# Linear attention and two expert layers on one core: an opening program of its own for the first three chunks, with native fp32 products and the low parts of the weights on GpSimd

## The reference

```python
# r, k, v, w: 4 x 8 x 768 x 48
for t in range(S):
    cur = einsum('bhd,bhe->bhde', u[None] * kt, vt)
    y[:, :, t] = einsum('bhd,bhde->bhe', rt, state + cur)
    state = wt[:, :, :, None] * state + einsum('bhd,bhe->bhde', kt, vt)
x = y.transpose(0, 2, 1, 3).reshape(3072, 384)
# first expert, 384 -> 1024 -> 384
h = x @ w_in
e = exp(h - max(h)); sm = e / (sum(e) + 1e-09)
solu = h * sm
ln = (solu - mean(solu)) / sqrt(var(solu) + 1e-06) * g_ln
x = ln @ w_out
# second expert, 384 -> 2048 -> 384
h = x @ w_in2
out = maximum(0.01 * h, h) @ w_out2
```

## Time and profile before

| | us |
|---|---|
| median of 3 runs | 826.4 (826.23 to 827.62) |
| the profiled execution's own time | 825.48 |
| its span, first to last instruction | 823.7 |
| TensorE busy | 786.2 (95%) |
| VectorE busy | 521.3 (63%) |
| ScalarE busy | 338.8 (41%) |
| GpSimd busy | 196.7 (24%) |

### The profile page before, as it was taken

The page is one execution under the profiler, slowest core; times in us unless marked ns, Lnnn a source line. Parts: engine busy times, 40 slices in busy tenths (PEclk is TensorE's granted clock), DMA queues, the critical chain, the costliest instruction groups (busy, mean ns, idle before and its releaser), DMA issues.

```text
span 823.7 us, 11957 instructions
## 1 busy us (share of the span) xinstructions
PE 786.2 (95%) x4570; PEld 746.2 (91%) x4570; DVE 521.3 (63%) x1068; ACT 338.8 (41%) x652; POOL 196.7 (24%) x216
## 2 busy tenths in 40 slices
PE   2877999999999999999999999999999999999996
PEld 2655999999999999999999999999999999999996
DVE  7778776576575676667665765666765775553332
ACT  3335644344433444434434444335443444334332
POOL 4477823113111221121221131122131121000000
PEclk9976899999999999999999999999999999999999
DMA  7772211203202302203202122113112030000000
GB/s 193 248 228 58 58 30 29 58 2 87 58 1 58 87 1 58 58 1 88 58 1 58 28 61 58 29 29 87 29 30 58 1 87 30 1 1 29 1 0 32
DMA packets 18847, 43.50 MB, mean 53 GB/s; under 512 B 2272, under 2 KB 14688, under 8 KB 18400
## 3 DMA queue, kind: packets, MB, share of 16 engines
q1 hardware_dynamic: 14736, 33.24, 16.5%
q10 hardware_dynamic: 4048, 9.44, 3.3%
HBM read 37.95 MB, written 4.72 MB: 52 GB/s over the span
## 4 chain that ended last, share of the span: by engine, by line
PE 85%; DVE 0%; ACT 0%; issue 0%; ACTq 0%
PE BANKS L964 60%; PE MISC L964 21%; PE BANKS L1075 2%; PE MISC L994 1%; PE MISC L987 1%; DVE Rraw L863 0%; DVE RL L869 0%; ACT RH L633 0%; ACT Rraw L626 0%; DVE X2L L875 0%; ACT X2H L638 0%; ACT OUT L644 0%; DVE A L745 0%; DVE nmean L817 0%; ACTq L248 0%
## 5 line engine op out<-in xcount | busy, mean ns | idle before, releaser
L626 ACT ACTIVATE Rraw<-BANKS 128x384 f32<-128x384 f32 x128 | 62.9, 492 | 239.5 <-PE BANKS L964 237.8
L863 DVE TENSOR_TENSOR Rraw<-BANKS,Rraw 128x384 f32<-128x384 f32 x128 | 71.3, 557 | 133.5 <-ACT Rraw L626 133.0
L964 PE MATMUL BANKS<-RH,W4H 128*128 128x384 f32 x384 | 138.6, 361 | 0.9 <-DVE RL L869 0.8
L964 PE MATMUL BANKS<-X2H,W3H 128*128 128x384 f32 x384 | 130.4, 339 | 0.2 <-DVE X2L L875 0.2
L964 PE MATMUL BANKS<-X2L,W3H 128*128 128x384 f32 x384 | 129.1, 336 | 0.0
L964 PE MATMUL BANKS<-RL,W4H 128*128 128x384 f32 x384 | 129.1, 336 | 0.0
L964 PE MATMUL BANKS<-X2H,W3L 128*128 128x384 f32 x384 | 129.0, 336 | 0.0
L964 PE MATMUL BANKS<-RH,W4L 128*128 128x384 f32 x384 | 129.0, 336 | 0.0
L633 ACT ACTIVATE RH<-Rraw 128x384 fp32r<-128x384 f32 x128 | 67.1, 524 | 73.2 <-DVE Rraw L863 73.2
L436 POOL TENSOR_TENSOR ke<-att 112x512 f32<-112x512 f32 x24 | 29.5, 1230 | 255.3 <-DVE att L739 255.3
L735 DVE RECIPROCAL ki<-att 112x128 f32<-112x128 f32 x96 | 90.1, 941 | 0.0
(11 more groups left out here) (117 smaller groups left out, 1509.3 us busy)
## 6 DMA issues: line engine op xcount, KB each, us to landing
att<-rkw SPq DMA_DIRECT2D x48, 288.0 KB, 4.9
rtok<-r_tok SPq DMA_DIRECT2D x24, 192.0 KB, 4.5
ktok<-k_tok SPq DMA_DIRECT2D x24, 192.0 KB, 4.6
vtok<-v_tok SPq DMA_DIRECT2D x24, 192.0 KB, 4.7
out<-OUT SPq DMA_DIRECT2D x8, 576.0 KB, 5.6
W3raw<-w_in ACTq DMA_DIRECT2D x1, 3072.0 KB, 11.2
W4raw<-w_out ACTq DMA_DIRECT2D x1, 3072.0 KB, 24.3
W1raw<-w_in ACTq DMA_DIRECT2D x1, 1536.0 KB, 9.5
```

Of the source, the lines that this page charges most:

```text
L626: nc.scalar.activation(Rraw[:, fp % 2, :], PR[fp % 2][:, 0:ST], ACT.Copy, scale=0.01).then_inc(act_slope, 1)
L863: nc.vector.tensor_tensor(Rraw[:, fp % 2, :], PR[fp % 2][:, 0:ST], Rraw[:, fp % 2, :], ALU.max).then_inc(dve_relu, 1)
L964: return nc.tensor.matmul(dst, lhsT, rhs, start=start, stop=stop, skip_group_check=True)
```

## The change

- Three chunks get a program of their own, written out engine by engine; LEAD stays 28, but only 24 items (chunks 0 to 2) run ahead of the second expert's first stage. Items 25 to 52 are spread over that stage's 16 steps (1 or 2 a step); before, its steps carried items 37 to 52.
- Inputs of chunks 0 to 2 are loaded at once: chunk 2's into `att2`, tokens of chunks 1 and 2 into `tok12`, chunk 2's masked scores into `A2`, all in the space of W4H, which is not filled yet. ScalarE issues the loads of W1, W3, W2 at once and W4 after chunk 2's keys.
- The first expert of these chunks is computed in native fp32: X (ScalarE's copy alone) by W1raw, six products of 512 columns a chunk; its second half as W2raw by the transposed rows, which ScalarE copies with the gain as scale, 24 products of 128 columns a chunk, chunk by chunk. The GpSimd multiplication of W2 by the gain is gone; in later M1 steps the gain is the scale of ScalarE's high part and of VectorE's RL.
- Masks are made for two pairs at once; keys and queries of chunk 0 are handed over in two halves. The floor of the scan is read from PSUM for these chunks. VectorE and GpSimd share the first clearing of `att`.
- All low parts are made by GpSimd, in groups of 768 columns (4, 4, 8 and 8 groups for W1 to W4); W3 and the first group of W4 in the opening, the rest of W4, W1 and W2 in the first stage of the second expert. TensorE waits for each group of W3 and W4 by itself, for W1 at chunk 3's expert, for W2 at the second M1.

```diff
-def batch_steps(last):
+def batch_steps(last, opening=False):
...
+    for k, so, f, fp in out:
+        if opening and fp <= STEPS:
+            done = [CPS * SLOTS + (F1 + LEAD - CPS * SLOTS + F2) * j // F2 for j in (f, f + 1)]
+        else:
+            done = [fp + LEAD - 1, fp + LEAD]
+        listed.append((k, so, f, fp, [slot_of(i) for i in range(done[0] + 1, done[1] + 1)]))
...
+            load_T(0, 0)
             load_tok(0, 0)
             sp.dma_start(ub[:, :], u.partition_broadcast(CH)).then_inc(ld_u, 16)
-            load_T(0, 1)
-            for i in range(1, LEAD + 1):
-                item(0, *slot_of(i))
...
+            for m in (1, 2):
+                load_T(0, m)
+                load_tok(0, m)
+            load_tok(0, 3)
+            load_T(0, 4)
+            load_T(0, 3)
...
+            def low_part(w, g):
+                pool.wait_ge(split_hi[w], g + 1)
+                if w == 0:
+                    pool.wait_ge(pe_h, 2 * CPS)
+                if w == 1:
+                    pool.wait_ge(pe_cons, F1)
+                nc.gpsimd.tensor_tensor(group(los[w], w, g), group(raws[w], w, g),
+                                        group(his[w], w, g).bitcast(F32), ALU.subtract).then_inc(split_lo[w], 1)
...
             def body(b, last, item=item):
...
+                    if opening(b, kind, so):
+                        if f % 2 == 0 and f // 2 + 1 < GROUPS[3]:
+                            low_part(3, f // 2 + 1)
+                        if f < GROUPS[0]:
+                            low_part(0, f)
+                        if F1 <= f < F1 + GROUPS[1]:
+                            low_part(1, f - F1)
...
+            def take_ln(m):
+
+                wait(act, pe_m1, m)
+                for f in range(F1):
+                    wait(act, pe_lnT, m * 2 + f // 4 + 1)
+                    nc.scalar.activation(first_ln[:, f, :], ln_bank(m, f // 4)[:, f % 4 * CH:(f % 4 + 1) * CH],
+                                         ACT.Identity,
+                                         scale=gain[:, f:f + 1]).then_inc(act_lnT, 1)
...
+            take_x(0, 2)
+            normalise(0, 0)
+            exp_rows(0, 1)
+            take_ln(0)
+            normalise(0, 1)
+            exp_rows(0, 2)
+            for g in range(2, 4):
+                high_part(2, g)
+            take_ln(1)
+            normalise(0, 2)
+            for g in range(4, 6):
+                high_part(2, g)
+            part_heads(0, 3)
+            for g in range(6, 8):
+                high_part(2, g)
+            take_ln(2)
+            take_range(0, 3)
+            for g in range(2):
+                high_part(3, g)
+            take_x2(0, 0)
+            for g in range(4):
+                high_part(0, g)
...
+            def first_expert(m, halves=(0, 1)):
+
+                pe.wait_ge(act_x, m + 1)
...
+                for n in halves:
+                    for k in range(KM):
+                        last = mm(hidden(0, m)[:, n * 512:(n + 1) * 512], X[:, k, :], w1[:, k, n * 512:(n + 1) * 512],
+                                  k == 0, k == KM - 1)
+                    last.then_inc(pe_h, 1)
...
+            def first_out(m):
...
+                for f in range(F1):
+                    pe.wait_ge(act_lnT, m * F1 + f + 1)
+                    for k in range(KM):
+                        last = mm(ACC[k][:, m * CH:(m + 1) * CH], w2[:, f, k * 128:(k + 1) * 128], first_ln[:, f, :],
+                                  m == 0 and f == 0, f == F1 - 1)
...
+            first_scores(0, range(PAIRS))
+            first_attend(0, (0, 1))
+            first_keys(0)
+            first_attend(0, (2, 3))
+            first_state(0)
+            first_transposes(0)
+            first_expert(0, (0,))
+            first_scores(1, range(PAIRS))
+            first_keys(1)
+            first_attend(1, range(PAIRS))
+            first_state(1)
+            first_scores(2, range(PAIRS))
+            first_expert(0, (1,))
+            first_transposes(1)
+            first_keys(2)
+            first_attend(2, range(PAIRS))
+            first_state(2)
+            first_expert(1)
+            first_transposes(2)
+            first_rows(0)
+            first_expert(2)
+            first_out(0)
+            for m in (1, 2):
+                first_rows(m)
+                first_out(m)
```

More of the change, by code:

```diff
@@ L185, in build, with part, queries, keys @@
         plan["top"] = end
+        def part(x, b, m):
+            return att2[:, x, :, :] if first(b, m) and m == 2 else att[:, m % 2, x, :, :]
+        def queries(b, m):
+            return part(0, b, m)
+        def keys(b, m):
+            return part(1, b, m)
+        def decays(b, m):
+            return part(2, b, m)
+        def masked(b, m):
+            return A2 if first(b, m) and m == 2 else A
+        def tokens(x, b, m):
+            return tok12[m - 1][:, x, :] if first(b, m) and m > 0 else (rtok, ktok, vtok)[x][:, :]
         w1r = [t[:, :].rearrange("p (k n) -> p k n", k=KM) for t in (W1H, W1L)]
@@ L370, in body @@
             def body(b, last, item=item, first_row=0):
-                for kind, so, f, fp, m, s in batch_steps(last):
-                    item(b, m, s)
+                for kind, so, f, fp, items in batch_steps(last, isinstance(b, int) and b == 0):
+                    for m, s in items:
+                        item(b, m, s)
                     if kind == "M1" and f == 3:
@@ L1060, in item, with attend @@
                     transpose_y(b, m)
-                if s == 8 and not (first(b, m) and m < CPS - 1):
+                if s == 8:
                     expert_in(b, m)
+            def attend(b, m, a, at):
+                inter = m % CPB > 0
+                if inter:
+                    if a == 0:
+                        wait(pe, dve_state, states(b, m - 1))
+                    mm(Y[:, a * PC:(a + 1) * PC], queries(b, m)[:, a, :], state[:, a, :], a == 0, False)
+                for h in range(2):
+                    c = (2 * a + h) * D
+                    last = mm(Y[:, c:c + D], masked(b, m)[:, at, h, :], tokens(2, b, m)[:, c:c + D], not inter and a == 0 and h == 0, True)
+                return last
```

621 lines of the change are left out of this document (365 added, 256 removed).

## The result

The changed kernel takes 833.7 us (median of 4 runs, 831.9 to 834.6) where the kernel before took 826.3 in the same session (825.8 to 827.6): a ratio of 1.0084, with a 95% interval of 1.0063 to 1.0106. So it is 7.4 us slower, where 16.5 us less was forecast. Its profiled execution took 831.9 us, 829.4 of them span; the forecast span was 807.2.

The account below looks back on a forecast made before the run. After the opening only TensorE's own work was taken to count. Opening 79.4 + rest 710.5 + moved items 12.3 + stalls 5 = 807.2 us of span; with 1.8 and 0.9 added, 809.9, range 802 to 824.

Parts of the forecast that it names:

- its walk: Opening, chunks 0 to 2, step by step: first expert from 22.8 us, end at 76.0 before any clock fall.
- bounds 0 to 2.1, 0 taken: Opening, first W1 product: cost of W1 landing later because 1.8 MB of inputs compete with its load.
- the gap before the first LN rows: Opening, near 49 us: TensorE idles 1.7 us while ScalarE copies X and normalises chunk 0.
- the 3.4 us for one fall: Opening: one fall of the granted clock after gaps of 1.7 and 1.8 us; bounds 0 and 7.
- The first rival: Opening: the clock stays down under native fp32, 33 us of doubled work, giving 840; chance 0.13 with its partial form.
- The third rival: The packed stage costs nothing and no clock fall comes, giving 803.5; chance 0.08.
- the 5 us for stalls in the first W3/W4 stage: Second expert's first stage: unhidden ScalarE, row-maximum and W1 low-part delays, 5 us; bounds 2 and 12.
- 12.3: First W3/W4 stage: TensorE work postponed into it, chunk 3 at 9.5 us and chunk 4's slots 1 to 4 at 2.8.
- The second rival: VectorE bounds the first W3/W4 stage: 34 two-SBUF-input operations blocked 1.2 us each, 107 against 84 us, giving 828; chance 0.08.
- The two slow rows: Old trace, beside GpSimd: four scans 3.28 us instead of 1.37, a key product 3.13 instead of 0.69.
- The price of 1.9 to 2.4 us a hold: VectorE beside GpSimd: extra time of one blocked operation, read from slow scans and a slow key product.
- The fourth rival: W2 or W4 loads late behind tokens 3 and inputs 3, 4: about 7 us, giving 817; chance 0.08.

Follow-up runs that it names:

- the kernel with the extra products: Twelve items run alone ahead of the stage, half wait, W1's high parts at about 40 us, plus 28 extra TensorE products, against the changed kernel's packing: 821.78 us, ratio 0.9949.
- the first experiment: Changed kernel with TensorE's wait before slot 2's scores again for half of the exponential products, the rest before the attention: 834.25 us, ratio 1.010.
- the kernels with the twelve items alone: Changed kernel with items 25 to 36 run by themselves ahead of the stage, then one item a step: 829.49 us; with the half wait too, 826.17 us.
- the reordering that came nearest to it: Changed kernel with the same GpSimd subtractions placed ahead of its long waits: 830.2 us, ratio 1.0037.
- the kernel without the extra products: The 817.82 us kernel (twelve items alone, GpSimd's subtractions moved away from VectorE's scans) with its 28 added TensorE products removed: 819.41 us, ratio 0.9911.

## Why the prediction was wrong

**The opening kept close to its walk, and ended 6.0 us early.** TensorE waited 2.11 us for W1 (bounds 0 to 2.1, 0 taken), but chunk 0 was quicker than walked, and the first W1 product came at 21.9 instead of 22.8. Six 512-column fp32 products took 5.3 us a chunk (5.2 forecast), 24 of 128 columns 5.5 (5.3 forecast, the value chosen from bounds of 0.20 and 0.30), the gap before the first LN rows was 1.71 (1.7). The granted clock was 1.00 from 40 us to the first W3 product, with no fall at either gap, so the 3.4 us for one fall weren't spent, and the first W3 product came at 74.45, where the sum puts it at 80.4. More than half of the 6.0 us gained here is that term of the clock, a choice between two bounds that fell the lucky way.

**The first rival fell.** The clock had risen to 1.00 by 28 us with native fp32 products alone before it, and dense streams of 512 and 128 columns ran at 1.00 for 34 us. What ran at 0.50 in the experiments was small attention work with gaps, as in the earlier trace rows. The third rival was half right: no fall came in the opening, but the packed stage cost far more than nothing.

**The step that failed is the 5 us for stalls in the first W3/W4 stage** (bounds 2 to 12). Its length was put at 64.9 + 12.3 + 5 = 82.2 us and was 104.7: 22.5 us too little. (The prediction has other figures for the same stage, 84.4 us of TensorE work under the splits and 90 us of length among its signs; the sum doesn't use them, and the 90 is too short as well.) In the sum a hold by GpSimd had no term of its own; it stood only as a rival. By the runs:

- 9.1 us go when GpSimd reads nothing for the low parts while it is even longer at work (104.74 to 95.65). This is the hold by the subtractions: the wait of 5.3 us, and some 3.5 for the 6.9 us at half clock around its end (an estimate from the waits and the clock above).
- 3.5 more go when GpSimd is also shorter at work (92.16). This is mostly the fall of the clock near 82, which hangs on half a microsecond of a wait; RL held up by token products is seen beside it, and that it is what makes the difference isn't tested alone.
- 9.9 stay: 10.2 us of idle time where 5 was allowed, in single waits of 1 to 2 us (masks behind statistics and row maximum, XL, LN), and TensorE busy 82.0 us at a clock of 1.00 where the sum counted 77.2 for the same work. They go only when the items are no longer packed: with one item a step the stage is 67.0 to 68.1 us. These stalls had been listed, each at about 1 us, and their number was too low.

**The second rival was the right mechanism at the wrong price, and with far too small a chance.** It named RL, scans and key products as the operations that GpSimd would hold, and gave 828; 833.7 came. In this stage only RL was held (scans stayed at 1.36 us for four, key products at 0.68); four scans were held in the kernel with the extra products. It was put at 0.08 on the ground that RL means 0.567 in steady stages "where GpSimd works beside it too". That row doesn't carry this, as the stretch of the first W3/W4 stage shows when it is read for GpSimd (after the length come TensorE, its weight loads, VectorE, ScalarE and GpSimd, each busy and count). In the kernel before:

```profile
114.25:179.19 64.94, 64.94 (x382) 62.75 (x382) 41.76 (x88) 26.33 (x52) 12.31 (x14) 1.00 0.15 37
```

In the changed kernel:

```profile
74.45:179.19 104.74, 87.82 (x472) 80.26 (x472) 67.68 (x131) 43.73 (x81) 51.54 (x43) 0.93 0.14 34
```

GpSimd's neighbourly work of the earlier trace rows is 12.3 us in 64.9, token, key and query steps without one weight subtraction; in the new stage it is 51.5 in 104.7, and 28 of these are subtractions of 1.8 us in runs. The two slow rows stood in the prediction, the scans of 3.28 beside GpSimd's key and token products and the key product of 3.13 beside its weight subtractions, and should have outweighed the average. Beside the second stands, on GpSimd in the kernel before:

```profile
88.06 7.08 POOL L477 TENSOR_TENSOR W4L<-W4raw,W4H 128x1024 fp32r<-128x1024 f32 x3
```

The key product began at 92.56, inside the second of these three, and ended at 95.69, 0.5 us behind the third: the length of a hold by a gapless run could be seen before the change. The price of 1.9 to 2.4 us a hold came from runs that ended soon after. The price was wrong in form as well: not 34 operations by 1.2 us, but RL's 16 by 0.44 on average, 7 us of VectorE time, and VectorE didn't become the bound (busy 67.7 of 104.7 us, close to the 66 counted). What cost most is one hold of 5.6 us, in an engine whose queue is in order, ahead of a mask for which TensorE has no other work. An average of busy time can't show that; the prediction asked whether the engines fit "as averages" and took yes for an answer.

The Trainium skill (SBUF — State Buffer, section SBUF: two separate sides) says that whichever starts first, a VectorE operation with two SBUF inputs or a GpSimd operation that reads SBUF, has the shared ports "for the whole instruction". The clears, which read nothing, agree with its condition (RL means 612 and 581 ns beside them, 1008 beside subtractions). The length of the hold goes beyond it: RL started at 147.57 and waited out not one GpSimd instruction but the remainder of one and three more that followed it without a gap.

**The rest was 5.7 us longer than 644.5.** 2.9 of it is an edit that the prediction overlooked, the wait before slot 2's scores (the first experiment); about 1.6 is the fall of the clock behind a wait of 2.2 us for chunk 5's normalised rows at the second M1, a wait that the kernels with the twelve items alone don't have; 1.2 is not placed.

Together: 6.0 less, 22.5 and 5.7 more, 22.2 in all, is the distance from 807.2 to 829.4.

The fourth rival (a late load) didn't happen: behind W1 no load ended a wait of TensorE in the opening's rows above. One of the prediction's signs for being wrong, more than 12 us of waits on VectorE in the stage, came out at 11.4 by name and 3.5 more under "issue", which stand before masks too.

## What to carry to other kernels

Before work is moved to GpSimd, list what VectorE does at the same time: an operation that reads two SBUF tiles can stand until GpSimd's whole run of reading operations is over, so such work belongs where VectorE has no SBUF-only operation that somebody waits for, or where TensorE has work to cover it (4.14 us of hold cost nothing with one item a step). That single pieces with gaps are better is argued from the lengths of the holds; the reordering that came nearest to it gained 3.5 us. Price a moved job from rows with the same neighbour, not from the mean of a stage where that neighbour is absent, and ask of a packed stage not whether the busy times fit but whether every hand-over is covered by the matmuls in front of it. A short wait of TensorE among small products may cost twice, since its clock can fall behind it (waits of 2.05 and 5.26 us in the changed kernel); the kernel without the extra products warns that curing the wait alone need not keep the clock up.

## What the hardware showed that was not expected

- A VectorE subtraction of 0.5 to 0.6 us took 5.58 us, until the end of a gapless run of GpSimd operations (8.01 and 4.14 in two other kernels); inside 11 us of GpSimd work that was mostly clears it took 0.50. Reciprocals (0.94) and masks (0.4, one input in PSUM) kept their times beside subtractions.
- Dense native fp32 products of 128 and 512 columns held the granted clock at 1.00 for 34 us, and a gap of 1.7 us among them didn't lower it; small attention products ran at 0.50 for over 9 us behind a wait of 3.2 us, and in another kernel for 13 us with no wait over 0.95 us before it.
- 24 native fp32 products of 128 columns take 5.5 us, 0.23 each; twelve records (six products) of 512 columns 5.3 us, 0.89 each.
